# Attention products with the values made for two query blocks at a time, in every second slot

## The chip, the cores and the metric

The kernel runs on one core of one Trainium2 chip. The metric is the device time of one execution in microseconds (us). The kernel before takes 2056.64 us, the median of 3 runs (2056.17 to 2059.11).

## The reference

Windowed causal attention with 4 batches of 8 heads, 576 positions and head size 64 is followed by two feed-forward layers. Cut to what matters:

```python
def _attn_ref(q, k, v):                       # 4 x 8 x 576 x 64
    scores = scale * q @ k.T
    mask = (rel >= 0) & (rel < 128)
    scores = where(mask, scores + bias, -1e9)
    attn = exp(scores - max); attn /= sum + 1e-9
    return attn @ v

x = attn_out.transpose(0, 2, 1, 3).reshape(2304, 512)
x = relu(x @ w_in) ** 2 @ w_out               # d_ff 2048
P = sinkhorn(x @ w_gate)                      # 8 experts
out = sum_e P[:, e] * (relu(x @ w1[e]) @ w2[e])
```

## The kernel before

**Stages.** The attention of batch 0 runs alone (to about 48 us). Then come four windows, one for each batch: window w computes the first feed-forward layer pair of batch w, and among its matmuls stands the attention of batch w+1 (there is none left for the last window). After that the expert stage runs to the end. This text is about the attention of batches 1 to 3, in the windows from about 52 to 446 us.

**The attention's tiles.** A batch has 20 blocks (`STEPS`): 4 pairs of heads (`KC`, index c) by 5 tiles of queries (`QT`, index t = block mod 5). A tile has 128 queries, the fifth (t = 4) has 64. A block looks at two tiles of keys, the first block of a pair of heads (t = 0) at one.

**The slots.** A batch has 23 slots, numbered j from 0 to 22. In slot j, TensorE (PE) does up to three things, in this order: `scores` of block j (L710, 4 matmuls), `transpose_p` of block j-2 (L721, 4 transposes of the probabilities, 2 where t = 0), and `attend` of block j-3 (L736, 4 products with the values, 2 where t = 0; each runs as two matmuls in the trace, so 8 rows or 4). The lags are `PE_LAG` = 2 and `OUT_LAG` = 3. `window_events` puts slot j behind a matmul group of the feed-forward layers (`SLOT_AFTER`); a group is 12 matmuls of layer 1 (`layer1`, L745) or of layer 2 (`layer2_features`, L752), and 64 groups make a window. All engines walk the same list of events, so each does its part of a slot in its own program order.

**Shapes.** Scores, transposes and both layers use weights of 128 columns. The products of L736 use weights of 64 columns: head 0 writes partitions 0 to 63 of bank 2 (`o_ps`), head 1 partitions 64 to 127. Where the block has 64 queries (t = 4), its transposes use 64 rows of the array (64x128 weights).

**What follows the products.** ACT copies the transposed probabilities out of bank 1 (`p_copy`, tile pT, two buffers). After the products, `o_hi` on ACT writes the high part of the block's output to xr, and `o_lo` on DVE the rest (L1174). PE waits for that (`x_lo`, through `bank_wait`) before it writes o_ps again. In a slot DVE has the two biased score reductions (L1140) and the normalisation of block j-1 (L1167) ahead of `o_lo`. ACT has two exponentials (L944), `p_copy`, `o_hi`. Semaphores: `pT_done`, `pT_out`, `pv_done`, `x_hi`, `x_lo`. SP waits on `pv_done` before it loads the values of another pair of heads. The first layer of a window waits on `x_lo`, and its relu on ACT (L1018) reads one of two banks.

Of the kernel before, what the change touches and what calls it, by code (L numbers as in the profile page):

```python
# [6 lines left out]
def attention_moe_moe_kernel(  # L7
# [22 lines left out]
    ALU = mybir.AluOpType  # L30
# [5 lines left out]
    E, _, F2 = moe2_w1.shape  # L36
    NTOK = B * S
    P = 128
# [8 lines left out]
    QT = -(-S // P)  # L47
    FULL = S // P
    TAIL = S - FULL * P
    STEPS = KC * QT  # L50
# [32 lines left out]
    with ctx:  # L83
        placed = {}

        def sb(name, shape, dt, at):

            size = 4
            for n in shape[1:]:
                size *= n  # L90
            tile = nc.alloc_sbuf_tensor_at(name, shape, dt, offset=BASE + at)
            placed[name] = at + -(-size // 32) * 32
            return tile

        def sem(name):
            return ctx.enter_context(nc.semaphore(name))
# [25 lines left out]
        v_sb = sb("v_sb", [P, 2, QT, 2 * D], fp32, placed["k_ll"])  # L122
        prob = sb("prob", [P, PB, 2, 2 * P], fp32, placed["v_sb"])
        pT = sb("pT", [P, 2, 2, 2, P], fp32, placed["prob"])
# [24 lines left out]
        at = W0  # L149
        for r in range(2):  # L150
# [4 lines left out]
            at = placed[f"a21_{r}"]  # L155
        assert at <= W0 + 2 * WS
        at = W0 + 2 * WS
        for r in range(2):
# [3 lines left out]
            at = placed[f"fl{r}"]  # L162
# [14 lines left out]
        o_ps = bank[2]  # L177
# [6 lines left out]
        def f(ap):  # L184

            return ap.bitcast(fp32)
# [24 lines left out]
        pv_done = sem("pv_done")  # L211
        x_hi = sem("x_hi")
        x_lo = sem("x_lo")
# [62 lines left out]
        def span(t):  # L276

            return (P if t < FULL else TAIL), (P if t == 0 else 0)

        def x_part(b, part, c, t, nq):  # L280

            at = slice(t * P, t * P + nq)
            return xr[:, bass.ds(b % 2, 1), part, c, at].rearrange("p o n -> p (o n)")

        PE_LAG, OUT_LAG = 2, 3
# [3 lines left out]

        def v_after(j):

# [74 lines left out]
        def bufs(b):  # L369

            return 2 if b == 0 else 1
# [304 lines left out]
        def _(pe):  # L676
# [10 lines left out]
            def bank_wait(what, b, j, n):  # L687

                if not isinstance(b, int) or j >= n:
                    wait_alone(pe, what, b * STEPS + (j - n + 1))  # L690
# [34 lines left out]
            def attend(b, j):  # L725

                c, t = j // QT, j % QT
                nq, k0 = span(t)
                if t == 0:
                    wait_alone(pe, v_in[c % 2], b * (3 * 16 * KC // 2) + 3 * 16 * (c // 2 + 1))  # L730
                bank_wait(x_lo, b, j, 1)
                wait_alone(pe, pT_out, b * STEPS + (j + 1))
                for kt in range(k0 // P, 2):
                    for h in range(2):
                        d = slice(h * D, (h + 1) * D)
                        last = pe.matmul(o_ps[d, 0:nq], v_sb[:, c % 2, t - 1 + kt, d], pT[:, j % 2, kt, h, 0:nq],  # L736
                                         start=(kt == k0 // P), stop=(kt == 1))
                last.then_inc(pv_done, 1)

# [17 lines left out]
            def stretch(events, w=None):  # L757

                for what, *a in events:
                    if what == "slot":  # L760
                        ba, j = a
                        n = bufs(ba)
                        if j < STEPS:
                            scores(ba, j, n)
                        if plain(ba) and j < STEPS:
                            rouse((0, 2, 4)[j] if j < 3 else 2)
                        if 0 <= j - PE_LAG < STEPS:
                            transpose_p(ba, j - PE_LAG, n)
                        if 0 <= j - OUT_LAG < STEPS:
                            attend(ba, j - OUT_LAG)  # L770
                    if what == "l1":
                        i, c = a
                        g = w * NB1 + i
                        if i < 2 and c == 0:
                            pe.wait_ge(x_lo, w * STEPS + (STEPS if i else STEPS - QT + -(-BH // P)))
                        if i % 2 == 0 and c == 0:
                            pe.wait_ge(w_split, w * (U1 * PIECES) + (i // 2 * PIECES + KC))
                        if g == 0 and c == 1:
                            pe.wait_ge(pT_out, STEPS - 1)
                        pe.wait_ge(relu_done, g * FC + (c + 1))  # L780
                        at = slice(i % 2 * BH, (i % 2 + 1) * BH)
                        layer1([xr[:, bass.ds(w % 2, 1), part, :, at].rearrange("p o c n -> p (o c) n") for part in (0, 1)],
                               slice(0, BH), BH, i // 2 % 2, c, l1_ps[c % 2])
                    if what == "l2":
                        i, m = a
                        g = w * NB1 + i
                        ys = y_banks(w)
                        if i % 2 == 0 and m == 0:
                            pe.wait_ge(w_split, w * (U1 * PIECES) + (i // 2 * PIECES + PIECES))
                        for c in ((0, 1), (2,), (3,), ())[m]:  # L790
                            pe.wait_ge(g_lo, g * FC + (c + 1))
                            for mm in range(len(ys)):
                                if c == 0:
                                    pe.wait_ge(y_free, g * KC + (2 if i == 0 else mm + 3 - len(ys)))
                                layer2_features(g, i // 2 % 2, mm, c, ys)
                        if m == KC - 1 and m >= len(ys):
                            pe.wait_ge(y_free, g * KC + (m + 3 - len(ys)))
                            for c in range(FC):
                                layer2_features(g, i // 2 % 2, m, c, ys)
# [127 lines left out]
        def _(act):  # L927
            def copy(o, i, scale=1.0):
                return act.activation(o, i, ACT.Copy, scale=scale)  # L929
# [23 lines left out]
                ps = pT_ps[(j + 1) % n][:, :].rearrange("p (k h n) -> p k h n", h=2, k=2)  # L953
                copy(pT[:, j % 2, ks, :, 0:nq], ps[:, ks, :, 0:nq]).then_inc(pT_out, 1)

            def o_hi(b, j):
                c, t = j // QT, j % QT
                nq, _ = span(t)
                act.wait_ge(pv_done, b * STEPS + (j + 1))
                copy(x_part(b, 0, c, t, nq), o_ps[:, 0:nq]).then_inc(x_hi, 1)  # L960

            def piece_hi(uses, s, i):

# [28 lines left out]
            def stretch(events, n16, u0, w=None):  # L992

                for what, *a in events:
                    if what == "xs":
                        operands_hi(a[0], xw[:, T1:, :, :], a[1])
                    if what == "ew":
                        first_hi(a[0], a[0])
                    if what == "split":
                        split_hi(*a)  # L1000
                    if what == "slot":
                        b, j = a
                        if 0 <= j - 1 < STEPS:
                            exponentials(b, j - 1)
                        if 0 <= j - PE_LAG < STEPS:
                            p_copy(b, j - PE_LAG, bufs(b))
                        if 0 <= j - OUT_LAG < STEPS:
                            o_hi(b, j - OUT_LAG)
                    if what == "w" and w is not None:
                        i = a[0]  # L1010
                        piece_hi(n16 + (i // 2 + 1) * 16, (u0 + i // PIECES) % 2, i % PIECES)
                    if what == "l1":
                        i, c = a
                        g = w * NB1 + i
                        act.wait_ge(l1_done, g * FC + (c + 1))
                        if c >= 2:
                            act.wait_ge(g_lo, g * FC + (c - 1))
                        act.activation(relu[:, c % 2, :], l1_ps[c % 2][:, 0:BH], ACT.Relu).then_inc(relu_done, 1)  # L1018
                        if c:
                            square_hi(g, c - 1)  # L1020
                        if c == FC - 1:
                            square_hi(g, c)
# [89 lines left out]
        def _(dve):  # L1112
# [54 lines left out]
                        last = dve.tensor_scalar(p, p, inv[:, h:h + 1], None, ALU.mult)  # L1167
                    last.then_inc(norm_done, 1)

            def o_lo(b, j):  # L1170
                c, t = j // QT, j % QT
                nq, _ = span(t)
                dve.wait_ge(x_hi, b * STEPS + (j + 1))
                dve.tensor_tensor(x_part(b, 1, c, t, nq), o_ps[:, 0:nq], f(x_part(b, 0, c, t, nq)),  # L1174
                                  ALU.subtract).then_inc(x_lo, 1)

            def square_lo(g, c):
                dve.wait_ge(g_hi, g * FC + (c + 1))
# [11 lines left out]
            def stretch(events, w=None):  # L1190
                for what, *a in events:
                    if what == "split":
                        split_lo(*a)
                    if what == "slot":
                        b, j = a
                        if j - 1 < STEPS:
                            softmax(b, j, bufs(b))
                        if 0 <= j - OUT_LAG < STEPS:
                            o_lo(b, j - OUT_LAG)
                    if what == "l1":  # L1200
                        i, c = a
                        g = w * NB1 + i
# [7 lines left out]
                    if what == "l2":  # L1210
                        i, m = a
# [177 lines left out]
```

## Time and profile before

| what | us |
|---|---|
| median of 3 runs | 2056.64 |
| the profiled execution's own time | 2056.02 |
| its span, first to last instruction | 2054.2 |
| PE busy in it | 2044.0 |
| DVE, ACT, POOL busy | 1291.0, 813.9, 1267.8 |
| L736, products with the values: 576 matmuls, last at | 444.0 |

The span is what the trace covers. Busy time of PE is a sum over matmuls whose ends are modelled, so a busy PE isn't one without gaps; start times of neighbouring matmuls tell the step between them. PEld is the load of weights, a row of its own. The granted TensorE clock is 1.000 over the whole span, the 2.4 GHz level.

### The profile page before, as it was taken

What the parts mean: (1) busy time and instruction counts of PE and PEld (TensorE: products, weight loads), DVE (VectorE), ACT (ScalarE), POOL (GpSimd) and SP (SyncE); (2) the same over time, 40 slices, a digit from 0 to 9 for tenths busy, and PEclk for the clock granted to TensorE, in tenths of its full rate; (3) what the DMA queues carried; (4) which work ended last, traced back from release to release, by engine and by line L of the source; (5) the groups of instructions that cost most, each with busy time, mean ns of one, the idle gap of its engine ahead of it and who ended that gap; (6) DMA issues with size and microseconds to landing.
All of it is one profiled execution on the core that took longest, in us unless ns stands there. A gap on an engine that the chain in (4) does not pass through costs nothing.

```text
span 2054.2 us, 36005 instructions
## 1 busy us (share of the span) xinstructions
PE 2044.0 (100%) x11896; PEld 1866.0 (91%) x11896; DVE 1291.0 (63%) x2687; ACT 813.9 (40%) x1607; POOL 1267.8 (62%) x1773
## 2 busy tenths in 40 slices
PE   8999999999999999999999999999999999999999
PEld 6999999999989989989989999998998998998998
DVE  8776766756486655655675555565566565556555
ACT  7665666645324323323343332332333333333331
POOL 5433334346476676677876666667777676676663
PEclk9999999999999999999999999999999999999999
DMA  5544433323212222222232222221223222222221
GB/s 151 128 107 114 114 101 104 97 68 82 68 52 72 69 65 71 64 69 71 63 103 63 71 71 61 71 71 62 71 68 97 72 61 71 67 65 71 63 71 62
DMA packets 178082, 161.47 MB, mean 79 GB/s; under 512 B 28992, under 2 KB 127808, under 8 KB 177984
## 3 DMA queue, kind: packets, MB, share of 16 engines
q1 hardware_dynamic: 177696, 159.93, 27.3%
q8 instruction: 54, 0.88, 0.2%
q14 instruction: 44, 0.36, 0.1%
q10 hardware_dynamic: 288, 0.30, 0.0%
HBM read 155.47 MB, written 4.72 MB: 78 GB/s over the span
## 4 chain that ended last, share of the span: by engine, by line
PE 97%; DVE 2%; ACT 1%; issue 0%; DVEq 0%; ACTq 0%
PE bank L864 38%; PE bank L810 34%; PE bank L752 10%; PE bank L745 10%; PE bank L736 2%; PE bank L721 1%; PE bank L710 1%; ACT prob L944 0%; PE bank L680 0%; PE bank L706 0%; DVE prob L1167 0%; PE bank L884 0%; DVE gl L1289 0%; DVE z_sb L1328 0%; DVE relu L1205 0%
## 5 line engine op out<-in xcount | busy, mean ns | idle before, releaser
L634 POOL TENSOR_TENSOR el<-ew,eh 128x256 fp32r<-128x256 f32 x672 | 473.6, 742 | 294.2 <-ACT eh L929 294.2
L1337 DVE SCALAR_TENSOR_TENSOR z_sb<-bank,gate,z_sb 128x512 f32<-128x512 f32 x540 | 403.9, 749 | 252.0 <-PE bank L864 252.0
L810 PE MATMUL bank<-xh,eh 128*128 128x384 f32 x1344 | 450.3, 335 | 0.0
L810 PE MATMUL bank<-xh,el 128*128 128x384 f32 x1344 | 450.2, 335 | 0.0
L864 PE MATMUL bank<-fh,gl 128*128 128x512 f32 x1152 | 450.1, 391 | 0.0
L864 PE MATMUL bank<-fl,gh 128*128 128x512 f32 x1152 | 449.9, 391 | 0.0
L810 PE MATMUL bank<-xl,eh 128*128 128x384 f32 x1344 | 449.6, 335 | 0.0
L864 PE MATMUL bank<-fh,gh 128*128 128x512 f32 x1152 | 449.1, 390 | 0.4 <-DVE z_sb L1328 0.4
L562 POOL TENSOR_TENSOR wl<-stage,wh 128x256 fp32r<-128x256 f32 x256 | 198.7, 797 | 291.0 <-ACT wh L929 290.3
L644 POOL TENSOR_TENSOR fl<-fw,fh 128x256 fp32r<-128x256 f32 x384 | 276.0, 752 | 136.1 <-ACT fh L929 135.8
L929 ACT ACTIVATE p<-bank 128x384 f32<-128x384 f32 x96 | 47.2, 492 | 669.0 <-PE bank L810 669.0
L864 PEld LDWEIGHTS bank<-fh,gl 128*128 128x128 f32 x1152 | 216.2, 188 | 45.3
L864 PEld LDWEIGHTS bank<-fh,gh 128*128 128x128 f32 x1152 | 216.3, 188 | 43.8 <-DVE z_sb L1337 0.6
L810 PEld LDWEIGHTS bank<-xh,eh 128*128 128x128 f32 x1344 | 252.3, 188 | 4.2 <-issue 0.5
L810 PEld LDWEIGHTS bank<-xl,eh 128*128 128x128 f32 x1344 | 252.3, 188 | 3.7
L864 PEld LDWEIGHTS bank<-fl,gh 128*128 128x128 f32 x1152 | 216.2, 188 | 43.0
L810 PEld LDWEIGHTS bank<-xh,el 128*128 128x128 f32 x1344 | 252.2, 188 | 0.0
L1289 DVE SCALAR_TENSOR_TENSOR gl<-bank,gh 128x384 fp32r<-128x384 f32 x384 | 203.7, 552 | 66.3 <-ACT gh L1055 55.3
L745 PE MATMUL bank<-xr,wh 128*128 128x288 f32 x1024 | 208.7, 298 | 0.0
L929 ACT ACTIVATE eh<-ew 128x1792 fp32r<-128x1792 f32 x96 | 162.8, 1696 | 12.6 <-POOL ew L627 12.6
L745 PEld LDWEIGHTS bank<-xr,wh 128*128 128x128 f32 x1024 | 163.8, 188 | 3.8 <-issue 3.3
L752 PE MATMUL bank<-g1h,wh 128*128 128x288 f32 x512 | 156.2, 305 | 0.5 <-DVE g1l L1179 0.5
(115 smaller groups left out, 2935.2 us busy)
## 6 DMA issues: line engine op xcount, KB each, us to landing
fw<-in_moe_w_dram SPq DMA_DIRECT2D x96, 512.0 KB, 3.7
ew<-in_moe_w_dram SPq DMA_DIRECT2D x96, 256.0 KB, 2.8
stage<-in_moe_w_in_dram SPq DMA_DIRECT2D x64, 256.0 KB, 2.9
stage<-in_moe_w_out_dram SPq DMA_DIRECT2D x64, 256.0 KB, 2.6
a<-in_moe_w_dram SPq DMA_DIRECT2D x96, 128.0 KB, 2.6
ew<-in_moe_w_dram SPq DMA_DIRECT2D x96, 128.0 KB, 2.8
acc<-in_k_dram SPq DMA_DIRECT2D x24, 288.0 KB, 4.5
acc<-in_q_dram SPq DMA_DIRECT2D x24, 288.0 KB, 4.8
```

Source lines behind the costliest of these rows:

```text
L562: last = pool.tensor_tensor(wl[s][:, i, at], stage[:, i % 2, at], f(wh[s][:, i, at]), ALU.subtract)
L634: last = pool.tensor_tensor(el[r][:, a, :, :], ew[r][:, a, :, :], f(eh[r][:, a, :, :]), ALU.subtract)
L644: last = pool.tensor_tensor(fl[r][:, c, at], fw[r][:, c, at], f(fh[r][:, c, at]), ALU.subtract)
L710: last = pe.matmul(s_ps[j % n][:, h * 2 * P + k0:(h + 1) * 2 * P], q_hl[:, c % 2, h, at], y[:, c % 2, h, keys], start=(y is k_hh), stop=(y ...
L736: last = pe.matmul(o_ps[d, 0:nq], v_sb[:, c % 2, t - 1 + kt, d], pT[:, j % 2, kt, h, 0:nq], start=(kt == k0 // P), stop=(kt == 1))
L745: last = pe.matmul(ps[:, 0:nt], w[s][:, kc, c * P:(c + 1) * P], xx[:, kc, at], start=(kc == 0 and w is wh and xx is hi), stop=(kc == KC - ...
L752: last = pe.matmul(ys[(g * KC + m) % len(ys)][:, 0:BH], w[s][:, KC + c, m * P:(m + 1) * P], x[:, c, :], start=(c == 0 and w is wh and x is ...
L810: done = pe.matmul(ps, w[r][:, a, kc, :], x[:, b, kc, :], start=(first and kc == 0 and w is eh and x is xh), stop=(kc == 1 and w is el), s ...
L864: done = pe.matmul(z_ps[t % 3][:, :], x[:, c, at], w[r][:, c, :], start=(c == 0 and x is ghf and w is fh), stop=(c == 1 and x is glf))
L929: return act.activation(o, i, ACT.Copy, scale=scale)
L1289: return dve.scalar_tensor_tensor(out=gl[:, r, f2, n2, :], in0=ps, scalar=0.0, in1=f(gh[:, r, f2, n2, :]), op0=ALU.max, op1=ALU.subtract)
L1337: dve.scalar_tensor_tensor(out=z, in0=ps, scalar=weight, in1=z, op0=ALU.mult, op1=ALU.add).then_inc(z_free, 1)
```

## The change

In batches 1 to 3 `attend` is no longer called in every slot. In slots with even j it is called for blocks j-4 and j-3, one after the other; in slots with odd j it isn't called. Block j-4 (even) writes columns 0 to 127 of o_ps, block j-3 (odd) columns 128 to 255. PE waits for `x_lo` once for the two. `transpose_p` moves behind `attend` on PE, and `p_copy` behind `o_hi` on ACT. `o_hi` and `o_lo` read both blocks in one instruction where they belong to the same pair of heads; where they don't (blocks 4 and 5, and 14 and 15), in two. In batch 0 the order and the lags stay; only the columns that an odd block uses differ.

```diff
+        def attended(b, j):
+
+            both = (j - OUT_LAG,) if b == 0 else (j - OUT_LAG - 1, j - OUT_LAG) if j % 2 == 0 else ()
+            return [n for n in both if 0 <= n < STEPS]
+
+        def read_out(b, j):
+
+            blocks = attended(b, j)
+            if len(blocks) == 2 and blocks[0] // QT == blocks[1] // QT:
+                return [blocks]
+            return [[n] for n in blocks]
+
+        def o_part(blocks, nq):
+
+            at = blocks[0] % 2 * P
+            return o_ps[:, at:at + nq]
...
-                bank_wait(x_lo, b, j, 1)
+                if b == 0:
+                    bank_wait(x_lo, b, j, 1)
+                elif j % 2 == 0:
+                    pe.wait_ge(x_lo, b * STEPS + j)
                 wait_alone(pe, pT_out, b * STEPS + (j + 1))
...
-                        last = pe.matmul(o_ps[d, 0:nq], v_sb[:, c % 2, t - 1 + kt, d], pT[:, j % 2, kt, h, 0:nq],
+                        last = pe.matmul(o_part([j], nq)[d, :], v_sb[:, c % 2, t - 1 + kt, d], pT[:, j % 2, kt, h, 0:nq],
...
-                        if 0 <= j - PE_LAG < STEPS:
+                        if ba == 0 and 0 <= j - PE_LAG < STEPS:
                             transpose_p(ba, j - PE_LAG, n)
-                        if 0 <= j - OUT_LAG < STEPS:
-                            attend(ba, j - OUT_LAG)
+                        for m in attended(ba, j):
+                            attend(ba, m)
+                        if ba and 0 <= j - PE_LAG < STEPS:
+                            transpose_p(ba, j - PE_LAG, n)
...
-            def o_hi(b, j):
-                c, t = j // QT, j % QT
-                nq, _ = span(t)
-                act.wait_ge(pv_done, b * STEPS + (j + 1))
-                copy(x_part(b, 0, c, t, nq), o_ps[:, 0:nq]).then_inc(x_hi, 1)
+            def o_hi(b, blocks, written):
+
+                c, t = blocks[0] // QT, blocks[0] % QT
+                nq = widths(blocks)
+                act.wait_ge(pv_done, b * STEPS + (written + 1))
+                copy(x_part(b, 0, c, t, nq), o_part(blocks, nq)).then_inc(x_hi, len(blocks))
...
-                        if 0 <= j - PE_LAG < STEPS:
+                        if b == 0 and 0 <= j - PE_LAG < STEPS:
                             p_copy(b, j - PE_LAG, bufs(b))
-                        if 0 <= j - OUT_LAG < STEPS:
-                            o_hi(b, j - OUT_LAG)
+                        for blocks in read_out(b, j):
+                            o_hi(b, blocks, attended(b, j)[-1])
+                        if b and 0 <= j - PE_LAG < STEPS:
+                            p_copy(b, j - PE_LAG, bufs(b))
```

`o_lo` on DVE changes in the same way as `o_hi`.

**PE, slots 3 and 4 of batch 2.** L710 are scores, L721 transposes, L736 products with the values, L745 and L752 the matmuls of the layers around them. Before:

```order
L710 MATMUL bank<-k_ll,q_hl 128x256
L721 MATMUL bank<-ident,prob 128x128 [waits pT_out,norm_done]
L721 MATMUL bank<-ident,prob 128x128 x3
L736 MATMUL bank<-pT,v_sb 64x128 [waits v_in0,pT_out]
L736 MATMUL bank<-pT,v_sb 64x128
L745 MATMUL bank<-xr,wh_50 128x288 [waits relu_done]
...
L710 MATMUL bank<-k_ll,q_hl 128x256
L721 MATMUL bank<-ident,prob 128x128 [waits pT_out,norm_done]
L721 MATMUL bank<-ident,prob 128x128 x3
L736 MATMUL bank<-pT,v_sb 64x128 [waits x_lo,pT_out]
L736 MATMUL bank<-pT,v_sb 64x128 x3
L752 MATMUL bank<-g1h,wh_50 128x288 [waits g_lo]
```

The same place after the change, where the lines L731, L742, L760, L769 and L776 are the former L710, L721, L736, L745 and L752:

```order
L731 MATMUL bank<-k_ll,q_hl 128x256
L742 MATMUL bank<-ident,prob 128x128 [waits pT_out,norm_done]
L742 MATMUL bank<-ident,prob 128x128 x3
...
L731 MATMUL bank<-k_ll,q_hl 128x256
L760 MATMUL bank<-pT,v_sb 64x128 [waits v_in0,x_lo,pT_out]
L760 MATMUL bank<-pT,v_sb 64x128
L760 MATMUL bank<-pT,v_sb 64x128 [waits pT_out]
L760 MATMUL bank<-pT,v_sb 64x128 x3
L742 MATMUL bank<-ident,prob 128x128 [waits pT_out,norm_done]
L742 MATMUL bank<-ident,prob 128x128 x3
L776 MATMUL bank<-g1h,wh_50 128x288 [waits g_lo]
```

Slot 3 has no products any more. Slot 4 has those of blocks 0 and 1, ahead of its transposes.

**ACT, slot 4 of batch 2.** Before (L944 exponentials, L929 copies; xr is `o_hi`, pT is `p_copy`):

```order
L944 ACTIVATE prob,psums<-prob,negmax 128x256
L929 ACTIVATE pT<-bank 128x512 [waits pv_done,pT_done]
L929 ACTIVATE xr<-bank 128x128 [waits pv_done]
L929 ACTIVATE q_hl<-acc 128x576 [waits q_in]
```

After:

```order
L970 ACTIVATE prob,psums<-prob,negmax 128x256
L955 ACTIVATE xr<-bank 128x256 [waits pv_done]
L955 ACTIVATE pT<-bank 128x512 [waits pv_done,pT_done]
L955 ACTIVATE q_hl<-acc 128x576 [waits q_in]
```

The two copies changed places, and the one to xr reads 256 columns.

## Rows read from the trace of the kernel before

**Rows 1.** The page: busy time (us, share, instructions), and the chain's shares by engine.

```profile
PE 2044.0 (100%) x11896; PEld 1866.0 (91%) x11896; DVE 1291.0 (63%) x2687; ACT 813.9 (40%) x1607; POOL 1267.8 (62%) x1773
PE 97%; DVE 2%; ACT 1%; issue 0%; DVEq 0%; ACTq 0%
```

**Rows 2.** Busy time by stretch: from score to score of batches 2 and 3.

```profile
185.77:318.63 132.86, 132.86 (x1067) 126.33 (x1065) 93.96 (x292) 81.62 (x232) 48.87 (x65) 1.00 0.41 109
318.63:451.50 132.87, 132.87 (x1067) 126.33 (x1066) 89.61 (x288) 79.55 (x228) 48.23 (x65) 1.00 0.35 91
```

**Rows 3.** Who waited for whom, PE and PEld, 46 to 552 us (total, times, longest).

```profile
PE bank L721 <- DVE prob L1167: 0.6, 1, 0.6
...
PEld bank L736 <- issue: 8.4, 50, 0.2
PEld bank L752 <- issue: 5.1, 30, 0.2
```

**Rows 4.** Timeline of PE, slot 4 of batch 2 (start, length in us; count last).

```profile
207.04 0.30 PE L752 MATMUL bank<-g1h,wl 128*128 128x288 f32 x1
207.18 0.28 PE L710 MATMUL bank<-k_hh,q_hl 128*128 128x256 f32 x1
...
207.65 0.60 PE L721 MATMUL bank<-ident,prob 128*128 128x128 f32 x4
208.18 0.66 PE L736 MATMUL bank<-pT,v_sb 128*64 128x128 f32 x8
...
209.00 0.30 PE L752 MATMUL bank<-g1l,wh 128*128 128x288 f32 x1
```

**Rows 5.** Timeline of the weight loads (PEld) in the same slot.

```profile
208.18 0.42 PEld L736 LDWEIGHTS bank<-pT,v_sb 128*64 128x64 f32 x8 [0.17 <-issue]
208.76 0.19 PEld L752 LDWEIGHTS bank<-g1h,wh 128*128 128x128 f32 x1 [0.17 <-issue]
```

**Rows 6.** PE by form over the whole span: busy us, mean ns of one.

```profile
L736 PE MATMUL bank<-pT,v_sb 128*64 128x128 f32 x448 | 38.6, 287 | 0.0
L721 PE MATMUL bank<-ident,prob 128*128 128x128 f32 x224 | 35.3, 274 | 2.9 <-DVE prob L1167 2.7
...
L736 PE MATMUL bank<-pT,v_sb 128*64 128x64 f32 x128 | 7.2, 234 | 0.0
```

**Rows 7.** Timeline of PE, slot 2 of batch 1: scores and transposes without products.

```profile
62.65 0.28 PE L710 MATMUL bank<-k_hh,q_hl 128*128 128x256 f32 x1
...
63.12 0.38 PE L721 MATMUL bank<-ident,prob 128*128 128x128 f32 x2
...
63.47 0.29 PE L752 MATMUL bank<-g1l,wh 128*128 128x288 f32 x1
```

**Rows 8.** Timeline of PE, slot 22 of batch 1: products of a 64-query block alone.

```profile
177.91 0.29 PE L752 MATMUL bank<-g1h,wl 128*128 128x288 f32 x1
178.13 0.45 PE L736 MATMUL bank<-pT,v_sb 128*64 128x64 f32 x8
...
178.75 0.30 PE L752 MATMUL bank<-g1l,wh 128*128 128x288 f32 x1
```

**Rows 9.** PE, slot 21 of batch 1: transposes of a 64-query block, then products.

```profile
171.15 0.29 PE L745 MATMUL bank<-xr,wl 128*128 128x288 f32 x1
171.37 0.46 PE L721 MATMUL bank<-ident,prob 64*128 64x64 f32 x4
171.76 0.66 PE L736 MATMUL bank<-pT,v_sb 128*64 128x128 f32 x8
172.34 0.54 PE L745 MATMUL bank<-xr,wh 128*128 128x288 f32 x2
172.72 0.30 PE L745 MATMUL bank<-xr,wl 128*128 128x288 f32 x1
```

**Rows 10.** Timeline of ACT, end of slot 6 of batch 2 (scores began at 217.65).

```profile
219.53 0.27 ACT L929 ACTIVATE xr<-bank 128x128 fp32r<-128x128 f32 x1
221.08 0.41 ACT L1018 ACTIVATE relu<-bank 128x288 f32<-128x288 f32 x1 [1.28 <-PE bank L745]
```

More of the change, by code:

```diff
@@ L278, in span, with widths @@
             return (P if t < FULL else TAIL), (P if t == 0 else 0)
+        def widths(blocks):
+            return sum(span(j % QT)[0] for j in blocks)
         def x_part(b, part, c, t, nq):
@@ L1168, in softmax, with o_lo @@
                     last.then_inc(norm_done, 1)
[L1170 to L1175, printed above, removed]
+            def o_lo(b, blocks, written):
+                c, t = blocks[0] // QT, blocks[0] % QT
+                nq = widths(blocks)
+                dve.wait_ge(x_hi, b * STEPS + (written + 1))
+                dve.tensor_tensor(x_part(b, 1, c, t, nq), o_part(blocks, nq), f(x_part(b, 0, c, t, nq)),
+                                  ALU.subtract).then_inc(x_lo, len(blocks))
             def square_lo(g, c):
@@ L1197, in stretch @@
                             softmax(b, j, bufs(b))
-                        if 0 <= j - OUT_LAG < STEPS:
-                            o_lo(b, j - OUT_LAG)
+                        for blocks in read_out(b, j):
+                            o_lo(b, blocks, attended(b, j)[-1])
                     if what == "l1":
```

## The prediction

> **What bounds the kernel now.** I read the page's busy times and its chain first. PE is busy for 2044.0 of 2054.2 us and carries 97% of the chain, DVE 2%, ACT 1% [rows 1]. The change touches only the attention of batches 1 to 3, so I looked at that stretch by windows: in batches 2 and 3, from first score to first score, PE is busy for all of 132.86 and 132.87 us, at a granted clock of 1.00, while DVE is busy for 94 and 90 and ACT for 82 and 80 [rows 2]. The waits of PE in the four windows agree: the largest on another engine is 0.6 us, once [rows 3]. So nothing that another engine saves counts here. Only a shorter stream of matmuls does, and the change keeps every matmul. What it can change is the time between them.
>
> That time shows among the weight loads. PEld stood idle 50 times before L736, 8.4 us in all, with nothing to wait for, and 30 times before L752, 5.1 us [rows 3]: 0.17 us each. In slot 4 of batch 2 one such gap stands before the first load of the products and one behind the last [rows 5]. The timeline of PE gives their price in steps between matmul starts. An ordinary step of the layers is 0.13 us (207.04 to 207.18 [rows 4]).
>
> - **Slot with two gaps.** From the first score (207.18) to the second layer matmul behind the slot (209.00) are 1.82 us; less one ordinary step, 1.69 [rows 4]. In it: scores 0.47 (to 207.65). Transposes: four in 0.60 us with 0.274 for the last, so (0.60 - 0.274) / 3 = 0.11 a step, 0.43 to 0.44 for four. Products: eight in 0.66 with 0.287 for the last, so 0.053 a step, 0.43 for eight [rows 4, 6]. Together 1.34. **0.35 is left for two switches, 0.175 each.**
> - **Slot without products.** 62.65 to 63.47 is 0.82, less a step 0.69; scores 0.47 and two transposes 0.22 make 0.69 [rows 7]. Nothing is left: going from scores to transposes and from transposes to a layer costs about 0.
> - **Products alone.** 177.91 to 178.75 is 0.84, less two steps 0.58. Eight products of 64 columns, in 0.45 with 0.234 for the last, at 0.03 a step are 0.25 [rows 6, 8]. 0.33 is left, again two switches, 0.165 each.
> - **Transposes of a 64-query block** use 64 rows of the array. 171.15 to 172.72 is 1.57, less three steps 1.17. Products 0.43, transposes 0.2 to 0.3 [rows 9]. 0.44 to 0.54 is left for what I count as three switches (into the transposes, into the products, out of them): 0.15 to 0.18 each.
>
> So a change in the shape of the array (128 columns to 64, or 128 rows to 64, and back) costs 0.15 to 0.18 us. I take 0.175, from the case that occurs most.
>
> A rule of the Trainium skill (page "TensorEngine Tiling (Array Packing)", section "Key Properties") says that changing the tiling mode, not just the tile, drains TensorE. It would put the price on every change of mode that the new order has, as I do below for pairs of neighbours that no row here shows.
>
> **The change, part by part.**
>
> *Switches on PE.* Before, 20 slots of a batch (3 to 22) have products: 2 switches each, 40, and one more in the four slots where the transposes are of a 64-query block (6, 11, 16, 21), 44. After, the 10 even slots from 4 to 22 have products: 20 switches. The 64-row transposes follow products in slots 6 and 16 and meet a layer behind them: one more each, 2. In slots 11 and 21 they stand without products and are entered and left: 4. Together 26. That is 18 fewer a batch, 54 in three batches, times 0.175: **-9.5 us**.
>
> *Neighbours that no row shows.* Scores to products (27 times), products to 128-row transposes (27). The nearest rows are layer to products and products to layer [rows 8], of the same shapes; I take 0.175. Bounds: 0, and the two switches' 0.35. I keep to one side of them, since 0 for 54 switches would contradict rows 8, in which the same shapes cost 0.33 for a pair. 64-row transposes to a layer (12 times): between 0 [rows 7] and 0.175 [rows 9]; I take 0.175, and 0 would give 2.1 us more.
>
> *The second block of a pair.* Its products have the first one's shape and follow at once, with one more wait (pT_out) in front. From scores to transposes costs nothing, with one wait in between in rows 7 and with two in rows 4 (the scores take 0.47 in both), so I take 0. The upper bound is a switch, 0.175 in 30 slots, 5.3 us.
>
> *Waits.* 30 waits on x_lo with their increments go. No row shows time for them: 0. Who waits now: PE, in an even slot, for the copy of block j-3, made in the odd slot before. That slot now ends earlier by its products and two switches, and the products stand ahead of the transposes; but a slot is followed by at least two groups of 12 steps, 3.1 us. Cover enough: 0. x_lo is now asked for once in two slots, so later than before.
>
> *ACT and DVE.* 24 fewer copies on ACT of about 0.27 [rows 10], and as many subtractions on DVE, at 8 in a batch; the wide ones are longer, so it comes to a few us. ACT waits 1.28 us for PE right behind such a slot [rows 10]: off the path, 0. In an even slot ACT waits for both blocks' products (1.7 us after the slot's start), then for the transposes, and ends at about 2.8 instead of the 2.15 of rows 10. The relu behind it isn't due before PE's next group ends, at 2.1 + 1.6 = 3.7. Cover of about 0.9; if it went, PE would wait at the layer.
>
> *SP.* Its loads of values wait for a block's products. For the third pair of heads this is block 4, done in slot 8 instead of 7; the next use is slot 14. Behind it in SP's queue stands a load of weights for which SP must wait for POOL's split anyhow. 0.
>
> *Sum.* The profiled execution took 2056.02, of which 2054.2 are its span. 2056.0 - 9.5 = 2046.5. The median of the runs is 0.6 above it, so I forecast **2047.1 us**.
>
> **The rivals.** A measurement can tell 0.2% here, 4.1 us.
>
> *A: the wait causes the gap, not the shape.* Every call of attend has waits in front. Then each block keeps its own entry and only the 30 exits are saved, less the 6 switches that the 64-row transposes add: 24 x 0.175 = 4.2, so 2052.4. For it: L736 has a wait each time. Against it: transposes have waits too and no gap ahead of them [rows 4, 7], and the gap behind the products stands before a layer whose like costs nothing elsewhere. Chance 0.07.
>
> *B: the slot becomes lumpy and PE waits.* The even slot is longer, the odd one shorter, and what PE saves it gives back in part at layers waiting for relu or g_lo. Five to nine us back: 2052.5 to 2056.5. Against it: the waits of rows 3 and the cover of 0.9. Chance 0.07.
>
> *C: slower.* The same place, with a price beyond the gain. ACT would have to finish its even slot more than 0.9 us later than I work out, and PE lose over (9.5 + 4.1) / 30 = 0.45 us at the layer behind each of the 30 even slots. At 0.6 us each it is 18.0 - 9.5, so 2065. It decides from 0.45. DVE, busy for 70% of the stretch, is the one that could hold ACT. Chance 0.04.
>
> *D: nothing.* If any load waited for the matmul before it whatever the shapes, grouping would save nothing: 2056.6. Rows 4 and 5 speak against it: loads of 0.19 us follow at steps of 0.13, so they run beside matmuls of the same rows. The Trainium skill (page "TensorE: Matmul & The Clock Gate", section "Measured speedup vs the span model") states that a load overlaps matmuls in flight only when the row group differs. By that rule the steps of the layers could not be 0.13; the trace here disagrees with it. Chance 0.02.
>
> **How the numbers follow.** The forecast has 0.80: 54 switches at 0.15 to 0.18 are 8.1 to 9.7, and with the 12 free exits up to 11.8, so 2044.8 to 2048.5, point 2047.1. The range takes in rival A at its top and is 2044.6 to 2052.4. Faster by over 0.2%: forecast and A, 0.87. Within: B and D, 0.09. Slower: C, 0.04.
>
> **What the changed profile would show.** Odd slots without any load gap (but in 11 and 21), and 0.91 us long instead of 1.48 to 1.70; even slots with two, of 0.17, and 1.9 to 2.1 us long; none between the two blocks' products. A batch from first score to first score of 129.7 instead of 132.86. The expert stage as long as before. Wrong would be: a gap between the two blocks (A), PE rows with waits on ACT or DVE behind even slots (B, C), or a batch still of 132.9 us (D).

## The result

The changed kernel takes **2046.45 us** (median of 6 runs, 2045.09 to 2046.98), the kernel before 2056.43 beside it (6 runs, 2055.82 to 2059.11). The ratio is 0.9949, 95% interval 0.9936 to 0.9962: 10.0 us faster. Forecast were 2047.1 us and faster by more than 0.2%.

**The profile after.** The profiled execution took 2046.91 us, its span 2045.1. The page's busy times and chain, to be read beside [rows 1]:

```profile
PE 2035.6 (100%) x11896; PEld 1866.3 (91%) x11896; DVE 1292.7 (63%) x2663; ACT 813.4 (40%) x1583; POOL 1264.8 (62%) x1773
PE 96%; DVE 2%; POOL 1%; ACT 1%; issue 0%; DMA 0%; DVEq 0%; ACTq 0%; SPq 0%
```

As many matmuls as before (11896), 8.4 us less PE time in the sum. DVE and ACT have 24 instructions fewer each and are as busy as they were. Busy time by stretch, batches 2 and 3 from first score to first score (to be read beside [rows 2]), and the four windows from the first matmul of a layer to the first of the experts. A line gives the stretch, its length, the busy time of PE, PEld, DVE, ACT and POOL with the number of instructions, the granted clock, the busy share of the DMA engines and their GB/s:

```profile
183.74:313.13 129.39, 129.39 (x1067) 125.97 (x1066) 94.02 (x284) 81.55 (x224) 48.44 (x65) 1.00 0.42 112
313.13:442.51 129.38, 129.38 (x1067) 125.96 (x1066) 90.17 (x280) 79.48 (x220) 48.04 (x65) 1.00 0.35 93
49.71:542.72 493.01, 491.92 (x3970) 480.41 (x3969) 337.36 (x956) 290.93 (x770) 211.21 (x275) 1.00 0.37 99
```

The same stretch of the kernel before:

```profile
48.25:551.61 503.36, 502.35 (x3971) 481.49 (x3969) 337.59 (x980) 291.04 (x794) 211.65 (x275) 1.00 0.37 97
```

A batch went from 132.86 to 129.39 us, 3.47 less, and the four windows from 503.36 to 493.01, 10.35 less. All of the gain is there. This execution began its first layer at 49.71 instead of 48.25. The profiled executions of the experiments, with the same batch 0, put it between 48.05 and 49.95, so batch 0's part varies as much from run to run, and the later start isn't put down to the change.

Timeline of PE in the changed kernel: slot 3 of batch 2 (transposes only), and slot 4 (products of two blocks, then transposes), the slot of [rows 4]:

```profile
198.09 0.28 PE L731 MATMUL bank<-k_hh,q_hl 128*128 128x256 f32 x1
...
198.57 0.60 PE L742 MATMUL bank<-ident,prob 128*128 128x128 f32 x4
198.92 0.51 PE L769 MATMUL bank<-xr,wh 128*128 128x288 f32 x2
...
204.59 0.28 PE L731 MATMUL bank<-k_hh,q_hl 128*128 128x256 f32 x1
...
205.15 0.88 PE L760 MATMUL bank<-pT,v_sb 128*64 128x128 f32 x12
205.96 0.66 PE L742 MATMUL bank<-ident,prob 128*128 128x128 f32 x4
206.37 0.38 PE L776 MATMUL bank<-g1h,wh 128*128 128x288 f32 x1
206.59 0.30 PE L776 MATMUL bank<-g1l,wh 128*128 128x288 f32 x1
```

The weight loads of slot 4, to be read beside [rows 5]:

```profile
204.82 0.19 PEld L731 LDWEIGHTS bank<-k_ll,q_hl 128*128 128x128 f32 x1
205.15 0.63 PEld L760 LDWEIGHTS bank<-pT,v_sb 128*64 128x64 f32 x12
205.95 0.42 PEld L742 LDWEIGHTS bank<-ident,prob 128*128 128x128 f32 x4 [0.17 <-issue]
```

Twelve products (four of block 0, eight of block 1) stand as one row: nothing separates the blocks. From the first score to the second layer matmul are 2.00 us, less an ordinary step 1.87. Scores 0.47, products 12 x 0.053 = 0.64 and transposes 0.44 make 1.55, so 0.32 is left for the two switches. Slot 3 is 0.92 us long by the same measure, its scores and transposes together 0.91, so nothing is left there. In its 64-query slots, too, the trace repeats what the prediction counted (slot 11, 64-row transposes alone: 1.06 us).

Who waited for whom, PE and PEld, 46 to 552 us (beside [rows 3]):

```profile
PE bank L742 <- DVE prob L1196: 1.3, 2, 0.7
...
PEld bank L742 <- issue: 6.3, 29, 0.9
PEld bank L760 <- issue: 1.3, 8, 0.2
```

Before the change this view had one more large group, the exits from products towards layer 1:

```profile
PEld bank L745 <- issue: 3.3, 19, 0.2
```

Over all its lines the view has 104 load gaps marked "issue" before and 40 now, most of them ahead of the transposes. It marks no gap under 0.15 us: the one ahead of products that follow scores is shorter (205.01 to 205.15 in the weight loads above) and isn't in it. So the marked gaps fell by more than the changes of shape did, which went from 132 to 78. The two waits for DVE's probabilities stand at 46.96 and 48.75, in batch 0, ahead of the windows.

ACT, the end of slot 6 of batch 2 (its scores began at 214.44; beside [rows 10]):

```profile
216.53 0.38 ACT L955 ACTIVATE pT<-bank 128x256 f32<-128x256 f32 x1
218.31 0.41 ACT L1047 ACTIVATE relu<-bank 128x288 f32<-128x288 f32 x1 [1.40 <-PE bank L769]
```

ACT is through with this even slot 2.47 us after its start and then waits 1.40 us for PE.

### The profile page after: what moved, and what is told of

The parts are those of the page before. It is cut to its first block, busy times and chain, and to the rows that moved or that the text cites. A ratio compares the mean times of both kernels' runs of the same rounds, so it can differ in the third digit from the quotient of the medians.

```text
span 2045.1 us, 35948 instructions
## 1 busy us (share of the span) xinstructions
PE 2035.6 (100%) x11896; PEld 1866.3 (91%) x11896; DVE 1292.7 (63%) x2663; ACT 813.4 (40%) x1583; POOL 1264.8 (62%) x1773
## 4 chain that ended last, share of the span: by engine, by line
PE 96%; DVE 2%; POOL 1%; ACT 1%; issue 0%; DMA 0%; DVEq 0%; ACTq 0%; SPq 0%
PE bank L890 38%; PE bank L836 34%; PE bank L776 9%; PE bank L769 9%; PE bank L742 2%; PE bank L760 2%; PE bank L731 1%; PE bank L727 1%; POOL xw L606 1%; PE bank L701 0%; POOL wl L583 0%; DVE prob L1196 0%; PE bank L910 0%; DVE gl L1319 0%; DVE z_sb L1358 0%
## 5 line engine op out<-in xcount | busy, mean ns | idle before, releaser
L769 PE MATMUL bank<-xr,wh 128*128 128x288 f32 x1024 | 208.4, 297 | 0.1
L769 PEld LDWEIGHTS bank<-xr,wh 128*128 128x128 f32 x1024 | 164.0, 189 | 1.0 <-ACT relu L1047 0.4
L776 PE MATMUL bank<-g1h,wh 128*128 128x288 f32 x512 | 155.5, 304 | 0.5 <-DVE g1l L1209 0.5
```

Of the source, the lines that this page charges most:

```text
L769: last = pe.matmul(ps[:, 0:nt], w[s][:, kc, c * P:(c + 1) * P], xx[:, kc, at], start=(kc == 0 and w is wh and xx is hi), stop=(kc == KC - ...
L776: last = pe.matmul(ys[(g * KC + m) % len(ys)][:, 0:BH], w[s][:, KC + c, m * P:(m + 1) * P], x[:, c, :], start=(c == 0 and w is wh and x is ...
```

## The experiments

No kernel leaves work out. "Windows" is the time from the first layer matmul to the first expert matmul in each profiled execution; it leaves the varying start out. The ratios are to the kernel before as it was measured beside each run: 2056.43 us for the change, 2056.76 for the first four experiments of the table, 2056.96 for the next three, 2056.39 for the last two.

| kernel | median us | ratio to before, interval | windows us |
|---|---|---|---|
| before | 2056.43 | | 503.36 |
| the change | 2046.45 | 0.9949 (0.9936 to 0.9962) | 493.01 |
| order_only | 2053.85 | 0.9986 (0.9976 to 0.9995) | 500.88 |
| split_pair | 2053.51 | 0.9985 (0.9976 to 0.9994) | 501.00 |
| more_waits | 2045.64 | 0.9944 (0.9929 to 0.9959) | 493.13 |
| threes | 2043.18 | 0.9935 (0.9922 to 0.9949) | 490.78 |
| products_first | 2057.78 | 1.0003 (0.9993 to 1.0012) | 504.07 |
| pairs_only | 2046.94 | 0.9956 (0.9942 to 0.9971) | 494.20 |
| narrow_reads | 2046.15 | 0.9946 (0.9929 to 0.9962) | 493.09 |
| threes_full | 2042.68 | 0.9932 (0.9919 to 0.9946) | 489.95 |
| threes_again | 2043.20 | 0.9934 (0.9921 to 0.9948) | 490.66 |

**order_only: the order inside a slot without the pairs.** The kernel before with:

```diff
-                        if 0 <= j - PE_LAG < STEPS:
+                        if ba == 0 and 0 <= j - PE_LAG < STEPS:
                             transpose_p(ba, j - PE_LAG, n)
                         if 0 <= j - OUT_LAG < STEPS:
                             attend(ba, j - OUT_LAG)
+                        if ba and 0 <= j - PE_LAG < STEPS:
+                            transpose_p(ba, j - PE_LAG, n)
```

and the same for `p_copy` and `o_hi` on ACT.

> The kernel before with only the order inside a slot changed: products with the values ahead of the transposes on PE, output copy ahead of the transposes' copy on ACT, still one block in every slot. Theory (the price is 0.175 us for each change of the array's shape): a batch keeps 44 such changes, so the same as before, 2056.4, within 1 us; a full slot is again 1.70 us long. Rival (the new order itself saves something, for instance because products of an earlier slot's copy never wait): up to 10 us faster, with gaps missing around L736.

It missed: 2053.85 us, windows 2.48 us shorter than before. The order has a gain of its own, smaller than the rival's, and not from missing gaps. Slot 4 of batch 2:

```profile
206.34 0.28 PE L710 MATMUL bank<-k_hh,q_hl 128*128 128x256 f32 x1
...
206.90 0.66 PE L736 MATMUL bank<-pT,v_sb 128*64 128x128 f32 x8
207.49 0.66 PE L721 MATMUL bank<-ident,prob 128*128 128x128 f32 x4
207.90 0.38 PE L752 MATMUL bank<-g1h,wh 128*128 128x288 f32 x1
208.12 0.29 PE L752 MATMUL bank<-g1l,wh 128*128 128x288 f32 x1
```

206.34 to 208.12, less a step, is 1.65, where [rows 4] gave 1.69. The other slots that have products and 128-row transposes are 0.05 shorter as well (0.07 in slots 10 and 15), those with 64-row ones aren't. 15 slots a batch at 0.05 are 2.3 us in three batches, nearly all of the 2.48.

**split_pair: the transposes between the two blocks' products.** The changed kernel with:

```diff
-                        for m in attended(ba, j):
+                        for m in attended(ba, j)[:1]:
                             attend(ba, m)
                         if ba and 0 <= j - PE_LAG < STEPS:
                             transpose_p(ba, j - PE_LAG, n)
+                        for m in attended(ba, j)[1:]:
+                            attend(ba, m)
```

> The changed kernel, but in even slots the transposes stand between the products of the two blocks. Same matmuls, same waits, same copies. Theory: 2 more changes of shape in 7 slots of a batch and 1 more in the two slots with transposes of a 64-query block, 16 a batch, 48 in all, times 0.175 is 8.4 us: 2054.8, with load gaps ahead of both blocks' products. Rival (a wait in front of a block's products makes the gap): each block's products have the same waits as in the changed kernel, so no new gap at the second block: 2046.4.

2053.51 us, and the windows 7.99 us longer than with the change; expected were 8.4. Weight loads in slot 4 of batch 2:

```profile
206.34 0.42 PEld L742 LDWEIGHTS bank<-ident,prob 128*128 128x128 f32 x4 [0.17 <-issue]
206.93 0.42 PEld L760 LDWEIGHTS bank<-pT,v_sb 128*64 128x64 f32 x8 [0.17 <-issue]
207.51 0.19 PEld L776 LDWEIGHTS bank<-g1h,wh 128*128 128x128 f32 x1 [0.17 <-issue]
```

The second block's products have the wait that they have in the changed kernel, and now a gap ahead of them. Two blocks at a time without being neighbours bring nothing over order_only (501.00 against 500.88). The count agrees: split_pair has 6 changes of shape fewer, about 1.0 us, but also 24 fewer of the exits towards 128-row transposes, which order_only showed to be 0.05 us cheaper, 1.2 us. This is the strongest run against the wait as the cause: matmuls, waits and copies are the same, only what stands beside what differs.

**more_waits: the wait repeated inside a block.**

```diff
                         d = slice(h * D, (h + 1) * D)
+                        if b and (kt, h) != (k0 // P, 0):
+                            wait_alone(pe, pT_out, b * STEPS + (j + 1))
```

> The changed kernel with the wait on the copied probabilities (and its increment) repeated ahead of each of a block's products but the first: 3 more for most blocks, 1 more for the first block of a pair of heads, 56 - 4 = 52 a batch, 156 in all, every one already satisfied. Theory (shape, not waits): 0, 2046.4 within 1 us. Rival (a wait costs PE a gap of 0.17): 156 x 0.17 = 27 us more, 2073; a small price for the sequencer would show as a step above 0.053 us between products.

2045.64 us, windows 493.13 against 493.01: nothing. PE by form over the whole span in this kernel:

```profile
L762 PE MATMUL bank<-pT,v_sb 128*64 128x128 f32 x448 | 34.4, 282 | 0.0
```

In the changed kernel the same products have 34.3 us and 282 ns. 156 satisfied waits with their increments cost 0.1 us at most here, under 1 ns each.

**threes: three blocks at a time.** The heart of the edit:

```diff
-            both = (j - OUT_LAG,) if b == 0 else (j - OUT_LAG - 1, j - OUT_LAG) if j % 2 == 0 else ()
-            return [n for n in both if 0 <= n < STEPS]
+            if b == 0:
+                return [n for n in (j - OUT_LAG,) if 0 <= n < STEPS]
+            first = (0, 3, 6, 9, 12, 14, 17, STEPS)
+            slots = (5, 8, 11, 14, 16, 19, 22)
+            return list(range(first[slots.index(j)], first[slots.index(j) + 1])) if j in slots else []
```

and three buffers of pT, 384 columns of o_ps, the third load of values one slot later, and small tiles of the expert stage moved to where they have room.

> Products for three blocks at a time: 7 slots of a batch (5, 8, 11, 14, 16, 19, 22), three buffers for the copied probabilities. Changes of shape a batch: 14 around products, 1 more in slots 11 and 16 each (64-query transposes next to products), 2 each in slots 6 and 21: 20 instead of 26. Theory: 18 fewer in all, times 0.175 is 3.2 us: 2043.3. Rival (longer slots give it back as waits of PE behind them): 2046.4 or more, with PE rows waiting for ACT or DVE.

2043.18 us, and 2043.20 when it ran again (threes_again): the forecast total. The windows are only 2.2 to 2.4 us shorter than with the change, where 3.2 were expected, so a part of the agreement is the varying start. The largest wait of PE on another engine is 1.1 us, once, where the scores of the second pair of heads of batch 1 wait for their queries on DVE (0.5 with the change); none stands behind the longer slots. All waits of PE in the windows together are 0.3 to 0.4 us longer. Without them 18 changes fewer are worth 2.6 us, 0.14 to 0.15 each.

**products_first: where the 0.05 us come from.** order_only, with the products ahead of the scores too:

```diff
+                        if ba and 0 <= j - OUT_LAG < STEPS:
+                            attend(ba, j - OUT_LAG)
                         if j < STEPS:
                             scores(ba, j, n)
...
-                        if 0 <= j - OUT_LAG < STEPS:
+                        if ba == 0 and 0 <= j - OUT_LAG < STEPS:
                             attend(ba, j - OUT_LAG)
```

> The kernel order_only with the products ahead of the scores as well: products, scores, transposes, one block in every slot. The question is why products, transposes cost 0.30 us for two changes of shape where transposes, products cost 0.35. Theory L (after a change of shape nothing hides the first load of weights; that of a layer or of scores takes 188 ns, that of a transpose 139, so leaving the products towards transposes is 0.05 cheaper): here the products are left towards scores, 188 ns, so about 0.35 a slot again and 2056.4, no faster than before. Rival E (entering the products from transposes is what is dear): here they are entered from a layer, so 2053.9 as in order_only.

2057.78 us, windows 504.07. The gain of order_only is gone, and a little more. The expectation had missed one thing: in slots 6, 11 and 16 the 64-row transposes no longer touch the products, one more change of shape each (1.84 us instead of 1.65, nine times, 1.7 us). The weight loads of slot 4:

```profile
208.06 0.42 PEld L736 LDWEIGHTS bank<-pT,v_sb 128*64 128x64 f32 x8 [0.16 <-issue]
208.65 0.19 PEld L710 LDWEIGHTS bank<-k_hh,q_hl 128*128 128x128 f32 x1 [0.17 <-issue]
```

The gap is 0.17 towards scores as it is towards transposes; what differs is what follows. Here the second score starts 0.22 us after the first, where 0.12 is its step. From the layer matmul ahead of it, the slot is 1.70 us long, as before. Rival E falls. That the 0.05 are the difference of the exposed load (188 to 139 ns) fits the four orders that ran, but no run changed the length of a load by itself: it is the likeliest reading and isn't shown.

**pairs_only: the pairs in the old order.** The changed kernel with `transpose_p` and `p_copy` back in front.

> The changed kernel with the old order inside a slot: transposes ahead of the products, and the transposes' copy ahead of the output's; two blocks at a time as in the change. Theory: the same 26 changes of shape a batch as the change, but in 27 slots the products are left towards a layer, 0.05 us dearer each: 2046.4 + 1.4 = 2047.8. Rival (the gain needs the new order): clearly above 2049.

2046.94 us, the median of 5 runs that spread widely (2046.30 to 2053.67), so the windows decide: 494.20, that is 1.19 longer than with the change. Expected were 1.4 for 27 slots; the products meet 128-row transposes in 21, which makes 1.05. Nine tenths of the gain (9.16 of 10.35 us) need only the pairs.

**narrow_reads: every block read out by itself.**

```diff
-            if len(blocks) == 2 and blocks[0] // QT == blocks[1] // QT:
-                return [blocks]
             return [[n] for n in blocks]
```

> The changed kernel with every block read out by an instruction of its own on ACT and on DVE (24 more on each). Theory (neither engine is on the path here): 2046.4 within 1 us, with ACT busier by about 3 us. Rival (reading two blocks together is part of the gain): slower by 1 us or more.

2046.15 us, windows 493.09 against 493.01. Reading the output of two blocks together is worth nothing in time. ACT is busy for 0.4 us more between 46 and 550 us and DVE for 2.6, less on ACT than I had put.

**threes_full: 128 rows for the 64-query transposes.** threes with:

```diff
+                        rows = P if b and not attended(b, j + PE_LAG) else nq
-                        last = pe.transpose(ps[:, kt, h, 0:nq], prob_of(b, j)[0:nq, h, kt * P:(kt + 1) * P],
-                                            ident[0:nq, 0:nq])
+                        last = pe.transpose(ps[:, kt, h, 0:rows], prob_of(b, j)[0:rows, h, kt * P:(kt + 1) * P],
+                                            ident[0:rows, 0:rows])
```

> The kernel threes, but where the transposes of a 64-query block stand without products beside them (slots 6 and 21 of a batch, 6 times in all) they run over all 128 rows of the array; the 64 extra columns that come out are read by nobody. Theory (using 64 rows is a change of shape like using 64 columns): the slot goes from 1.06 us (two changes, four transposes at 0.06) to 0.90 (none, four at 0.11), without load gaps; 6 x 0.16 is 1.0 us: 2042.2. Rival (rows don't matter, the 64-row slots are long for another reason): four transposes 0.05 longer each, 1.2 us slower, 2044.4.

> The kernel threes once more on the same chip as threes_full, since their difference is expected to be 1 us. Theory: 2043.2, so 1.0 above threes_full. Rival: at or below threes_full.

2042.68 against 2043.20 us on the same chip. The ranges of the runs overlap (2042.28 to 2043.08, 2042.51 to 2044.23), so the time alone wouldn't settle it. The timeline of PE does. Slot 6 of batch 2, in threes_again:

```profile
214.24 0.28 PE L739 MATMUL bank<-k_hh,q_hl 128*128 128x256 f32 x1
...
214.81 0.46 PE L750 MATMUL bank<-ident,prob 64*128 64x64 f32 x4
215.19 0.54 PE L777 MATMUL bank<-xr,wh 128*128 128x288 f32 x2
215.57 0.30 PE L777 MATMUL bank<-xr,wl 128*128 128x288 f32 x1
```

and in threes_full:

```profile
213.05 0.28 PE L739 MATMUL bank<-k_hh,q_hl 128*128 128x256 f32 x1
...
213.53 0.60 PE L751 MATMUL bank<-ident,prob 128*128 128x128 f32 x4
213.88 0.51 PE L778 MATMUL bank<-xr,wh 128*128 128x288 f32 x2
214.23 0.30 PE L778 MATMUL bank<-xr,wl 128*128 128x288 f32 x1
```

From the first score to the third layer matmul, less two ordinary steps, 1.06 us became 0.91 (0.90 was expected), though each transpose is longer by itself. Slot 21 gains the same; six slots make 0.9, and the windows are 0.7 us shorter. Bank and source are the same in both, only the rows differ: using 64 rows costs a change of shape too. This is the fastest kernel of the study, 13.7 us below before.

**64 columns against 128.** No experiment isolates the columns. The products differ from their neighbours in a second thing besides their 64 columns, that each runs as two matmuls in the trace. The trace of the kernel before has a place that separates the two. Behind a layer of the experts stand five matmuls that transpose the gate logits, each again two in the trace, four with weights of 128 columns (L896) and one with 64 (L899), from the same source into the same bank:

```profile
567.14 0.33 PE L810 MATMUL bank<-xh,el 128*128 128x384 f32 x1
567.32 0.96 PE L896 MATMUL bank<-ident,lgs 128*128 128x16 f32 x8
568.21 0.29 PE L899 MATMUL bank<-ident,lgs 128*64 128x16 f32 x2
568.42 0.45 PE L810 MATMUL bank<-xh,eh 128*128 128x384 f32 x1
568.71 0.34 PE L810 MATMUL bank<-xl,eh 128*128 128x384 f32 x1
```

L896 comes 0.17 us behind the layer's matmul, the layer's own step: entering it costs nothing. The last L896 starts at 568.01, so the step to L899 is 0.19 where L896's own is 0.11, and the second L810 behind comes 0.17 later than steps of 0.08 and 0.17 would have it. That is 0.25 us for the pair of changes around 64 columns. Leaving a double matmul of 128 columns costs nothing either: L873 stands between L864 at 575.43 and the second L864 behind it at 576.11, 0.68 us, which is two steps of 0.23 and two of 0.11. So it is the columns. The second place with L899 (571.66), ahead of L864 instead of L810, gives 0.24, and the changed kernel's trace has the same steps. Both are less than the 0.35 around the products, so the price isn't one number for all neighbours; why it is lower here stays open.

## Why the prediction was right

- **What bounds:** PE in the windows, at a granted clock of 1.00, so that a gap on PE is lost time. Held: narrow_reads changed the work of ACT and DVE and not the time. (The wait of 0.6 us that the prediction took from [rows 3] stands at 47.29, ahead of the windows; inside them the longest was 0.5.)
- **The cause, shape and not waits:** held. Against waits stand split_pair (same waits, 8.0 us longer) and more_waits (156 more waits, 0.1 us), so rival A falls. For shape stand threes_full (rows) and L896 beside L899 in the trace (columns).
- **The count, 54 changes of shape:** held slot by slot. Odd slots of 1.48 to 1.72 us became 0.86 to 0.93 where four transposes use 128 rows; slots 7 and 17, with two transposes, which the prediction's figures leave out, went from 1.26 or 1.27 to 0.70. Even slots with products and scores have 1.66 to 2.09, where 1.9 to 2.1 was forecast. A batch takes 129.4 us where 129.7 were forecast. Two counts of neighbours were off, without effect on the sum at one price: scores meet products 24 times, not 27 (slot 20 has no scores), and products meet 128-row transposes 21 times, not 27 (in slots 6 and 16 they have 64 rows).
- **The price, 0.175 us:** a little high and not one number. The pairs alone (pairs_only against before) gave 9.16 us in the windows, 0.170 for each of the 54. Against order_only, the change gave 7.87, 0.146 each.
- **The order of products and transposes**, the term that was mis-sized: I put every neighbour that no row showed at the same 0.175. Products left towards 128-row transposes turned out 0.05 us cheaper. In the change that is 21 slots, about 1.1 us that the sum didn't have. The order is worth 1.19 us (pairs_only) and the pairs 9.16 instead of 9.5: together 10.35 in the windows, 10.0 between the medians. The two errors go opposite ways, so the forecast is a little nearer than its terms.
- **The covers:** held. ACT had 1.40 us to spare behind an even slot, where 0.9 was forecast. Inside the windows PE waits on other engines no longer than before (0.5 us for L731, as for L710 before, and 0.5 for L776, as for L752), so rivals B and C have nothing to stand on; D falls with the result. (B's five to nine us added to 2047.1 are 2052.1 to 2056.1, 0.4 below the figures given for it.) The second block's wait and SP's later load show no cost either.
- **The Trainium skill** (page "TensorEngine Tiling (Array Packing)", section "Key Properties"): a change of the tiling mode drains TensorE. The runs agree in that such a change costs time, for columns (gaps of 0.17 us in split_pair) and for rows (threes_full); that a drain is what fills the time they don't show. The rule of the Trainium skill weighed in rival D (page "TensorE: Matmul & The Clock Gate"; it stands in the section "The mechanism", not in the one that the prediction names) doesn't hold for the loads of this kernel, which are 0.19 us long and follow at steps of 0.13 over the same rows.

## What to carry to other kernels

On an engine that is busy all the time, look for gaps ahead of weight loads that wait for nothing ("issue"), and count where neighbouring matmuls use different parts of the array: in the slots of this kernel each such change cost 0.14 to 0.18 us, the work being the same, and about 0.12 around L899. Put matmuls of one shape next to each other, as many blocks as buffers and PSUM allow, and where a change must stay, try which neighbour makes it cheapest (here the transposes). Measure such a price from slot lengths at matmul starts, not from busy time, which hides it.

## What I had not expected

- The price of a pair of changes depends on what follows: 0.35 us towards layers and scores (weight loads of 188 ns), 0.30 towards transposes (139 ns). The length of the load as the reason isn't shown. Swapping two groups that both stay in the slot gave 2.5 us.
- A matmul group over all 128 rows with half of its output unused is faster than one over 64 rows, if it saves two changes: the slot took 0.91 against 1.06 us.
- The stretch before the first layer matmul varies by up to 1.9 us between executions (48.05 to 49.95), as much as several of the effects studied here, so small differences had to be read from the windows.
